# Routing by three fixed 24-bit rounds, slots placed with the test, and multiplies that fill TensorE's pauses

## Time and profile before

| | before |
|---|---|
| runs (us) | 956.94, 959.58, 955.23; median 956.94 |
| the profiled execution, its own time | 957.17 us |
| span of its records | 955.3 us |
| PE / DVE / ACT / POOL busy | 85 / 45 / 39 / 34% of the span |
| mean granted TensorE clock | 0.92 of full speed |

### The profile page before, as it was taken

How to read it: one execution, slowest core, us unless ns; L and a number is a source line. 1 busy time by engine, 2 the same in 40 slices (tenths; PEclk the granted TensorE clock), 3 DMA queues, 4 the chain that set the end, 5 groups by cost and what they waited for, 6 DMA issues and landing times.

```text
span 955.3 us, 15745 instructions
## 1 busy us (share of the span) xinstructions
PE 815.8 (85%) x5831; PEld 784.9 (82%) x5831; DVE 427.9 (45%) x833; ACT 375.5 (39%) x662; POOL 325.2 (34%) x245
## 2 busy tenths in 40 slices
PE   6999999602231199999999999999999999999996
PEld 5989898502221199999999999999999999999995
DVE  5777777386667414323423332332431432342331
ACT  4666666345444014323323332332432432332332
POOL 4677777360000216124324422512702612431001
PEclk9999999755555599999999999999999999999999
DMA  9999997211000002112110310301211111100000
GB/s 181 175 185 196 182 170 146 94 66 66 0 0 0 26 25 67 67 51 67 67 50 5 127 40 9 111 31 39 66 66 49 66 66 49 66 0 25 1 1 25
DMA packets 126802, 64.98 MB, mean 68 GB/s; under 512 B 102448, under 2 KB 119856, under 8 KB 126768
## 3 DMA queue, kind: packets, MB, share of 16 engines
q1 hardware_dynamic: 123696, 55.09, 25.6%
q0 software_dynamic: 3072, 9.44, 3.0%
HBM read 55.07 MB, written 9.44 MB: 68 GB/s over the span
## 4 chain that ended last, share of the span: by engine, by line
PE 82%; issue 8%; DVE 5%; ACT 2%; SPq 1%; DMA 1%; DVEq 1%; POOL 0%; ACTq 0%; POOLq 0%
PE psum L1291 21%; PE psum L1293 21%; PE psum L1292 21%; PE psum L1097 3%; PE psum L1149 3%; PE psum L1180 2%; PE psum L1195 2%; PE psum L1134 2%; PE psum L1249 2%; PE psum L1158 1%; PE psum L1188 1%; PE psum L1126 1%; PE psum L1301 1%; SPq L419 1%; ACT junk_a L722 1%
## 5 line engine op out<-in xcount | busy, mean ns | idle before, releaser
L1079 DVE SCALAR_TENSOR_TENSOR psum<-rg,psum 128x384 f32<-128x384 f32 x128 | 72.0, 563 | 155.3 <-ACT rg L756 155.3
L756 ACT ACTIVATE rg<-psum,three 128x384 f32<-128x384 f32 x128 | 74.5, 582 | 153.0 <-PE psum L1293 153.0
L1291 PE MATMUL psum<-yh,w_high 128*128 128x384 f32 x384 | 130.7, 340 | 0.9
L1291 PE MATMUL psum<-w_high,gh 128*128 128x384 f32 x384 | 128.4, 334 | 0.3 <-DVE gl L1082 0.3
L1293 PE MATMUL psum<-yh,w_low 128*128 128x384 f32 x384 | 128.5, 335 | 0.0
L1292 PE MATMUL psum<-yl,w_high 128*128 128x384 f32 x384 | 128.5, 335 | 0.0
L1293 PE MATMUL psum<-w_high,gl 128*128 128x384 f32 x384 | 128.3, 334 | 0.0
L1292 PE MATMUL psum<-w_low,gh 128*128 128x384 f32 x384 | 128.3, 334 | 0.0
L614 POOL DMA_INDIRECT out_dram<-ys,ids x24 | 24.0, 1001 | 256.8 <-ACT ys L771 252.2
L1069 DVE SCALAR_TENSOR_TENSOR hl<-psum,hh 128x384 fp32r<-128x384 f32 x64 | 35.7, 558 | 166.9 <-ACT hh L746 166.9
L1082 DVE SCALAR_TENSOR_TENSOR gl<-psum,gh 128x384 fp32r<-128x384 f32 x128 | 71.4, 558 | 72.4 <-ACT gh L760 72.4
(11 more groups left out here) (183 smaller groups left out, 1785.0 us busy)
## 6 DMA issues: line engine op xcount, KB each, us to landing
raw<-in_moe_w_dram SPq DMA_DIRECT2D x16, 1536.0 KB, 6.4
f_in<-in_f_logit_dram SPq DMA_DIRECT2D x24, 192.0 KB, 4.2
k_in<-in_k_dram SPq DMA_DIRECT2D x24, 192.0 KB, 4.7
q_in<-in_q_dram SPq DMA_DIRECT2D x24, 192.0 KB, 5.1
v_in<-in_v_dram SPq DMA_DIRECT2D x24, 192.0 KB, 4.3
x_rows<-x_nat SPq DMA_DIRECT2D x24, 192.0 KB, 3.9
raw<-in_moe_w_in_dram SPq DMA_DIRECT2D x12, 256.0 KB, 4.0
raw<-in_moe_w_out_dram SPq DMA_DIRECT2D x12, 256.0 KB, 3.1
```

Source lines behind the costliest of these rows:

```text
L756: act.activation(rg[:, j % 2, :], banks[j % 3][:, 0:CAP], ACT.Relu, bias=three[:, 0:1]).then_inc(r_done, 1)
L1079: dve.scalar_tensor_tensor(out=bank, in0=rg[:, j % 2, :], scalar=6.0, in1=bank, op0=ALU.min, op1=ALU.mult).then_inc(gg_done, 1)
L1291: pe.matmul(bank, high, rhs_high, start=start, stop=False)
```

## The change

Six things, all in the routing and the turn into the first expert.

- **Three rounds without a test, of 6 steps.** Rounds 0 to 2 are written out, not looped, and search 24 bits of the threshold (the low 8 bits are left zero); only after the third is `excess` looked at. Then the register loop runs at most seven passes of full 8-step rounds. The flag is read once behind each choice into a register that is kept, and a pass tests the register alone.
- **The split of the counting.** VectorE counts 11 tiles instead of 12, ScalarE 13 instead of 12. A quarter bank is left free between them, so that no bank is read by both.
- **Widening.** VectorE widens the first six tiles itself (two copies of three tiles), ScalarE the other 18 straight behind `vm`, without the flag.
- **Early slots.** The slot arithmetic moves into `judge`, behind each tested choice. One matrix `order` replaces `before`, `steps_to` replaces `tots` and `keep`, and a minimum over the experts replaces the multiply by `chb` and the sum. `parts` moves to ScalarE, and ScalarE makes 7 of the 24 one-hot tiles as relu(1 - |column - c|).
- **Gather.** Each of the three transfers has a semaphore, and TensorE transposes a tile when it has landed.
- **Multiplies into an unread bank.** `warm(n)` is n products of ones, 128x128 in bfloat16, into bank p0; `warm_late(n)` n float32 products of the identity. There are 40 before the first choice, 8 before the transposes of each untested choice, 6 behind the last step of each search, 16 behind each threshold, 16 behind the loop, 11 late ones behind the token numbers and 4 behind the first gathered tokens.

```diff
-ND = NTOK // 2
+ND = 11 * P
+COARSE = 3
+COARSE_STEPS = 6
@@ ScalarE
-            def widen_first(r):
-                act.wait_ge(v_made, r + 1)
-                widen(r, 0)
+            def widen_rest(r):
+                act.wait_ge(v_made, r + 1)
+                for part in range(1, 4):
+                    wide, narrow = widening(widened(part))
+                    act.copy(wide, narrow).then_inc(v_wide, 1)
...
+            act.wait_ge(placed, 1)
+            act.mul(parts[:, :, 0, :], in_block[:, :, :], lane[:, 0:1]).then_inc(parts_done, 1)
+            away = junk_a[:, 0:P * (NT - HOT_DVE)]
+            for n in range(HOT_DVE, NT):
+                done = act.activation(away[:, P * (n - HOT_DVE):P * (n - HOT_DVE) + P], columns[:, :], ACT.Abs, scale=-1.0,
+                                      bias=column_of[:, n:n + 1])
...
+            act.activation(in_column[:, HOT_DVE:NT, :].rearrange("p n c -> p (n c)"), away, ACT.Relu, scale=-1.0,
+                           bias=ones[:, 0:1]).then_inc(columns_done_too, 1)
@@ VectorE
+                for tiles in (slice(0, PART // 2), slice(PART // 2, PART)):
+                    wide, narrow = widening(tiles)
+                    dve.tensor_copy(wide, narrow).then_inc(v_wide_first, 1)
+
+            def judge(r):
...
+                dve.sem_inc(flag_ready, 1)
...
+                dve.tensor_tensor_scan(flat(incl[:, :, :]), flat(steps_to[:, :, :]), count_ps, 0.0, ALU.add,
+                                       ALU.subtract).then_inc(placing, 1)
...
+                dve.tensor_tensor(flat(incl[:, :, :]), flat(incl[:, :, :]), order_ps, ALU.add).then_inc(placing, 1)
+                placing_to(2)
+                dve.tensor_reduce(slotf[:, :], incl[:, :, :].rearrange("p e n -> p n e"), AX.X, ALU.min).then_inc(placing, 1)
+                placing_to(3)
+                dve.tensor_scalar(block_of[:, :], slotf[:, :], ROUND_TO, -ROUND_TO, ALU.add, ALU.add).then_inc(placing, 1)
...
+                load_flag(dve, over)
...
             choose(0)
-            with dve.Fori(0, ROUNDS) as r:
-                dve.engine_nop().then_inc(flag_ready, 1)
-                with dve.If(over_flag(dve) != 0):
-                    search(r)
+            for r in range(COARSE):
+                search(r, COARSE_STEPS, 0)
+            over = dve.alloc_register()
+            judge(COARSE)
+            with dve.Fori(COARSE, COARSE + ROUNDS) as r:
+                with dve.If_ne(over, 0):
+                    search(r, STEPS, SKIPPED)
+                    judge(r + 1)
                     dve.sem_inc(passed, 1)
...
+            dve.sem_inc(placed, 1)
+            for n in range(HOT_DVE):
@@ TensorE
+            def warm(count):
+                for i in range(count):
+                    pe.matmul(p0[:, P * (i % 4):P * (i % 4) + P], ones_b[:, :], ones_b[:, :], start=True, stop=True)
+
+            def warm_late(count):
+                for i in range(count):
+                    pe.matmul(p0[:, P * (i % 4):P * (i % 4) + P], ident[:, :], ident[:, :], start=True, stop=True)
...
+            def turn_choice(r):
+                pe.wait_ge(chosen, r + 1)
+                warm(8)
+                turn_values(r)
...
+                turn_values(r)
+                pe.wait_ge(flag_ready, r - COARSE + 1)
+                pe.sem_inc(passed, 1)
+                load_flag(pe, over)
+
+            def thresholds(r, steps, skipped):
+                for i in range(steps):
+                    pe.wait_ge(ok_ready, steps * r + i + 1 - skipped)
                     pe.matmul(digit_ps, group[:, :, :].rearrange("p a b -> p (a b)"), ok[:, :], start=True, stop=True).then_inc(n_ready, 1)
+                warm(6)
                 pe.wait_ge(t_known, r + 1)
                 pe.matmul(thr_ps, ones[:, :], thead[:, :], start=True, stop=True).then_inc(t_ready, 1)
-                count_choice(r + 1)
+                warm(16)
...
+            warm(40)
+            over = pe.alloc_register()
+            turn_choice(0)
+            for r in range(COARSE):
+                thresholds(r, COARSE_STEPS, 0)
+                if r < COARSE - 1:
+                    turn_choice(r + 1)
+            count_choice(COARSE)
+            with pe.Fori(COARSE, COARSE + ROUNDS) as r:
+                with pe.If_ne(over, 0):
+                    thresholds(r, STEPS, SKIPPED)
+                    count_choice(r + 1)
+            warm(16)
...
             done.then_inc(ids_summed, 1)
-
+            warm_late(11)
...
-            for c in range(3):
-                x_turn(0, c)
+            for t in range(3):
+                pe.wait_ge(xs_loaded[t], 16)
+                for c in range(3):
+                    last = pe.transpose(banks[x_bank(0, c)][:, P * t:P * t + P], xs[:, t, P * c:P * c + P], ident[:, :])
+                    if t == 2:
+                        last.then_inc(x_turned, 1)
+            warm_late(4)
```

More of the change, by code:

```diff
@@ L304, in build @@
         split_done = sem("split_done")
-        xs_loaded = sem("xs_loaded")
+        xs_loaded = [sem(f"xs_loaded{t}") for t in range(3)]
         x_turned = sem("x_turned")
@@ new lines, in count, with flag_known @@
+            def count(i, next_bits):
+                if i:
+                    act.wait_ge(bits_ready, next_bits)
+                key = bits if i else first_key
+                act.activation(junk_a[:, :], v_act, ACT.Sign, scale=-1.0, bias=key[:, 1:2].bitcast(F32),
+                               accum_out=count_a).then_inc(counted, 1)
+            def flag_known(r):
+                act.wait_ge(flag_ready, r - COARSE + 1)
+                act.sem_inc(passed, 1)
+                load_flag(act, over)
@@ L714, in search @@
+            widen_rest(0)
+            for r in range(COARSE):
+                act.wait_ge(v_turned, r + 1)
+                for i in range(COARSE_STEPS):
+                    count(i, (COARSE_STEPS - 1) * r + i)
+                widen_rest(r + 1)
             def search(r):
-                for part in range(1, 4):
-                    widen(r, part)
+                act.wait_ge(placing, PLACE * (r - COARSE) + 2)
                 act.wait_ge(v_turned, r + 1)
                 for i in range(STEPS):
[L719 to L730, removed]
-                    search(r)
+                    count(i, (STEPS - 1) * r + i - SKIPPED)
+                widen_rest(r + 1)
+                flag_known(r + 1)
+            over = act.alloc_register()
+            flag_known(COARSE)
+            with act.Fori(COARSE, COARSE + ROUNDS) as r:
+                with act.If_ne(over, 0):
+                    search(r)
@@ L1027, in _ @@
[L1027 to L1033, removed]
@@ L1041, in _ @@
[L1041 to L1046, removed]
@@ L1258, in search @@
-            def search(r):
-                for part in range(1, 4):
-                    last = turn_values(r, part)
-                last.then_inc(v_turned, 1)
-                for i in range(STEPS):
-                    pe.wait_ge(ok_ready, STEPS * r + i + 1)
+                pe.matmul(order_ps, order[:, :], chn[:, :, :].rearrange("p n e -> p e n"),
+                          start=True, stop=True).then_inc(order_counted, 1)
+                turn_values(r)
+                pe.wait_ge(flag_ready, r - COARSE + 1)
```

171 lines of the change are left out of this document (93 added, 78 removed).

## The result

The change makes the kernel faster: median 929.01 us (926.87 to 932.75, 4 runs) against 956.85 (955.23 to 959.58, 4 runs), ratio 0.971, 95% interval 0.967 to 0.9751. The forecast was 929.5. Run again in a later group, the same kernel had a median of 926.61 us (926.22 to 927.7, 4 runs), ratio 0.9693 (0.9677 to 0.971). The median of all eight runs is 927.3. The profiled execution took 927.81 us, its span is 926.1.

What follows compares the result with a forecast made beforehand. The half-speed routing, 177 to 334 us, was taken as bound by waits passing between VectorE and TensorE. Terms 15.8 + 3.1 + 4.7 - 1.0 + 1.3 + 1.6 + 0.7 + 0.7 + 1.2 - 0.4 = 27.7 gave 929.5 us, range 923.5 to 937.5.

Steps and rivals of the forecast that it cites:

- Rounds and steps: Searches: three short rounds and one full, 26 steps for 32, gain 15.8 us; counting split 11 to 13, gain 3.1.
- Turning: Second and third choice, chn to count: earlier widening and earlier clock rise gain 2.2 and 2.5 us, together 4.7.
- First choice: Ahead of the first count: 48 multiplies stand in the path, 5.1 us; transposes end at 189.6, loss 1.0.
- Fourth choice and last one: Fourth chn to count 5.7 us, gain 1.3; last chn to one-hot tiles 10.2 us, gain 1.6.
- One-hot tiles: Tiles shared by VectorE (17 in 2.8 us) and ScalarE (about 3.3): 3.8 us against 4.5, gain 0.7.
- Threshold behind six multiplies: Search end: multiplies finish about 0.1 us after `thead`, four times, 0.4 us lost.
- Gather and first expert: Only 3 transposes follow the last transfer, gain 0.7 us; first expert's products mostly escape half clock, gain 1.2.
- the clock stays low: Rival: multiplies and short bursts don't lift the routing's clock earlier; 937 us, chance 0.08.
- the multiplies stand in the way: Rival: each multiply costs 0.2 us instead of 0.11, adding 12; 942 us, chance 0.06.
- refetched code: Rival: TensorE's jumps over its grown loop body cost 5.1 us each, twice an empty pass; 989 us, chance 0.03.
- an extra taker: Rival: coarse thresholds leave an extra taker, forcing one more full round of 28.6 us; 958 us, chance 0.03.
- the rule of the Trainium skill: TensorE's clock: full clock does not engage for transposes, as they don't count as activity; the forecast held the trace disagrees.

Runs made afterwards that it cites:

- steps8: Changed kernel with the three untested rounds searching 32 bits in 8 steps again instead of 6; 945.58 us, ratio 0.9879.
- no_forty: Changed kernel without the 40 multiplies ahead of the first choice; 925.59 us, ratio 0.9681.
- no_fill: Changed kernel without any of the added multiplies, bfloat16 or float32; 930.59 us, ratio 0.972.
- no_warm: Changed kernel without the bfloat16 multiplies, the 15 late float32 ones kept; 928.73 us, ratio 0.9711.
- one_jump: Changed kernel with the first tested round written out and one jump over the loop instead of six empty passes; 923.24 us, ratio 0.9655.
- even_split: Changed kernel with VectorE and ScalarE counting 12 tiles each again; 932.37 us, ratio 0.974.

## Why the prediction was right, step by step

The total was right (27.7 forecast, 29.2 between the profiles, 27.8 between the first medians) and its mechanism too. The terms had errors of both signs, which partly cancelled: the total is nearer to the forecast than the single terms earn.

- **Rounds and steps.** Four rounds ran, three short and one full, as the stretches show: 26 steps. `steps8` prices the six steps at 15.1 us, at the new pitch of 2.52; I had taken 15.8 at the old pitch, which is right beside a split counted for 26 steps. The split gave 0.11 a step for 0.12. The searches gained 17.9 for 18.9. The split explains 0.3 of the difference. The rest are pauses for which the sum had no term: GpSimd's splits hold the first search up by 1.5 us where it was 1.2 before and the second by 0.2, and a pause of about 0.2 us stands before the last count of the third search, where VectorE starts later than ScalarE (249.54 against 249.32).
- **Turning.** 3.87 us where I had 4.45 in the third choice. Two things were sized too high: the two copies take 0.63 together, not 0.9, and TensorE's clock rose 4.1 us after it had become busy (229.6 to 233.7), not 5. In the other choices it was 4.3, 4.6, 5.2 and 6.0, so the term varies by up to half of these differences from choice to choice. In the second choice the sum of 5.7 was met by 5.85: stalls of 0.8 in `vm` and 1.4 in the copies, partly covered.
- **First choice.** Forecast 189.6, measured 189.01, of which 0.3 is the attention's earlier end; the 48 multiplies took 5.0 us for 5.1, and `no_forty` shows that the sign of this term was right: it is a loss the change makes itself.
- **Fourth choice and last one.** 5.2 for 5.7 and 9.4 for 10.2: the same too dear copies, and passes of 0.69 instead of 0.75. Of the second, 0.3 is a slip of the sum: the parts written there, 4.8 + 0.6 + 4.5, add up to 9.9.
- **One-hot tiles: the term that failed.** Forecast +0.7, measured 0. I had costed VectorE's 17 tiles at 2.8 us, the pitch of the old 24, and they took 3.78. The first of them lasted 1.18 us, while GpSimd made its half of `parts` (1.16 us), and ended with it (293.24 against 293.20). Before, VectorE's own `parts` had stood beside that operation (1.37 us) and had most likely been stalled by it; I had taken it away as if the stall went with it. No run moved GpSimd's half. ScalarE's share was too cheap as well, 3.90 us for about 3.3: its seven distances over 896 columns took 2.14 us where the one relu over the same number took 1.04, so a price by columns leaves out what each short operation costs by itself. The two engines ended together, at 295.9, and either alone would have held the last products.

```profile
L1103 DVE TENSOR_SCALAR in_column<-columns,column_of x17: 242/243/1181, 292.1 to 295.6; 128x128 bf16<-128x128 bf16 x17
```

(the group of the one-hot tiles in the changed kernel: duration in ns least, median, most.) The operations beside it:

```profile
291.99 0.78 ACT L764 ACTIVATE parts<-in_block,lane 128x576 bf16<-128x576 bf16 x1 [6.62 <-DVEq L1101]
292.04 1.16 POOL L621 TENSOR_TENSOR parts<-in_block,row_base 128x576 bf16<-128x576 bf16 x1 [74.64 <-DVEq L1101]
...
292.67 2.14 ACT L767 ACTIVATE junk_a<-columns,column_of 128x128 bf16<-128x128 bf16 x7
...
294.85 1.04 ACT L771 ACTIVATE in_column<-junk_a,ones 128x896 bf16<-128x896 bf16 x1
```

- **Threshold behind six multiplies.** No loss for a forecast 0.4: 2.65 us as before.
- **Gather and first expert.** 0.9 and 1.5 for 0.7 and 1.2; the first expert's products ran at full clock from their start in this execution.

Of the rivals, *the clock stays low* is excluded by the third choice and by its reverse in `no_fill`; *the multiplies stand in the way* holds for the first choice alone, at a pitch of 0.107 us at half clock, half the price that it needed; *refetched code* is excluded by VectorE's 0.69 us passes, by its 0.5 us jump, and by TensorE, which was through its own passes at 290.8, 1.3 us ahead of VectorE; but TensorE's 5.1 us behind the attention are still there (5.12 us, and 5.05 in `no_forty`), and no run here tried their cause; *an extra taker* did not occur.

The words of the change put the multiplies into its name; by the runs they are its small part. Of the 29.2 us 17.9 lie in the searches, and the multiplies are worth net 1.6 us by the medians and 4.2 by the profiles, a total that the runs do not settle.

## What to carry to other kernels

In this kernel filling TensorE's pauses paid where the real work behind the filler followed without a gap and was itself bound by TensorE (2.2 us in the third choice); where the work was waiting for TensorE already, as ahead of the first choice, the filler was a loss (1.8 us for 40 multiplies). Look for the second kind of place before adding any. When an operation is moved off an engine, ask whether its duration was its own or a stall that another engine caused: the stall stays and falls on what comes next. Count the empty passes of a guarded loop as work: at 0.7 us each, six cost more here than all the slot arithmetic (2.7 us from scan to `in_block`).

## What the runs showed of the hardware that was not expected

- Transposes of float32 against the identity lift TensorE's clock by themselves: in the kernel without multiplies the clock rose between 237 and 238 us, behind 4.8 us of transposes alone, and in `no_warm` at 208.6, behind 3.5 us of them. This goes against the rule of the Trainium skill ("TensorE: Matmul & The Clock Gate", Part 4) that the forecast weighed.
- The full clock can end at the worst place, at the first product of a long run (`one_jump`, 300.3 us, restored at 303.7), after TensorE had been busy 0.25 to 0.55 us of five of the six microseconds from 294 on, while the gathered tiles landed:

```profile
299.00:300.00 1.00, 0.26 (x3) 0.07 (x1) 1.00 (x3) 0.43 (x2) 0.83 (x1) 1.00 0.00 0
301.00:302.00 1.00, 1.00 (x5) 1.00 (x5) 0.00 (x0) 0.00 (x0) 0.70 (x2) 0.50 0.57 181
303.00:304.00 1.00, 1.00 (x5) 1.00 (x4) 0.00 (x0) 0.49 (x1) 0.00 (x0) 0.63 0.49 120
```

The late multiplies did not prevent it in three other kernels that hold them: in `steps8`, `even_split` and `no_warm` the clock had risen, fell before the first product, and was back 0.9 to 1.7 us after it (620.32, 619.93 and 620.05 us behind the first product, against 619.5 to 619.7 where it stayed full). What decides between the two, no run here shows.

- A VectorE operation on two integers per lane can last 1.1 us when GpSimd works beside it (0.15 alone), while its counts over 1408 PSUM columns never changed from 1.74 us.
